# Moving the pooled normalisation of five units to GpSimd in an attention and two-layer MLP kernel, with two roundings and eight feature sums made at other units

## What is computed

```python
# q, k, v: (4, 8, 576, 64)
q_d = q.reshape(B, H, 144, 4, D).mean(axis=3)        # k_d and v_d likewise: the pooled branch
out_d = softmax(scale * q_d @ k_d.T) @ v_d            # 144 x 144 per head
out_up = np.repeat(out_d, 4, axis=2)
mask = np.abs(pos[:, None] - pos[None, :]) < 4        # the band branch
out_local = softmax(where(mask, scale * q @ k.T, -1e9)) @ v
x = (out_up + out_local) -> (2304, 512)
h = x @ w_in;  x = (h * sigmoid(h)) @ w_out           # 512 -> 2048 -> 512
h = x @ w_in2; out = (h * sigmoid(1.702 * h)) @ w_out2
```

## Time and profile before

| | |
|---|---|
| median of 3 runs | 814.86 us (814.63 to 815.61) |
| the profiled execution | 815.39 us, its span 813.6 us |
| TensorE busy | 801.9 us, 99% of the span |
| VectorE, ScalarE, GpSimd busy | 654.1, 538.8, 192.5 us |
| granted TensorE clock | 1.000, full speed (2.4 GHz) |

### The profile page before, as it was taken

The page is one execution under the profiler, slowest core; times in us unless marked ns, Lnnn a source line. Parts: engine busy times, 40 slices in busy tenths (PEclk is TensorE's granted clock), DMA queues, the critical chain, the costliest instruction groups (busy, mean ns, idle before and its releaser), DMA issues.

```text
span 813.6 us, 15682 instructions
## 1 busy us (share of the span) xinstructions
PE 801.9 (99%) x5800; PEld 776.5 (95%) x5800; DVE 654.1 (80%) x944; ACT 538.8 (66%) x865; POOL 192.5 (24%) x199
## 2 busy tenths in 40 slices
PE   9999899999999999999999999999999999999998
PEld 5777699999999999999999999999999999999998
DVE  7999889999998767998768888899655688555466
ACT  5889776578745677655678555677455687455773
POOL 5789786720045420235300000000000000000000
PEclk9999999999999999999999999999999999999999
DMA  7887668776868797677887777878887778877873
GB/s 241 230 253 226 162 198 276 256 284 218 287 209 275 262 322 249 210 264 252 277 292 249 231 253 253 270 234 272 283 289 253 266 252 265 301 251 262 279 254 137
DMA packets 98331, 205.42 MB, mean 252 GB/s; under 512 B 8432, under 2 KB 56048, under 8 KB 98256
## 3 DMA queue, kind: packets, MB, share of 16 engines
q1 hardware_dynamic: 98256, 204.42, 76.5%
HBM read 160.87 MB, written 43.52 MB: 251 GB/s over the span
## 4 chain that ended last, share of the span: by engine, by line
PE 81%; POOL 8%; DVE 7%; issue 4%; ACT 0%; POOLq 0%; DVEq 0%; ACTq 0%
PE hid L330 42%; PE yp L356 36%; DVE gr L547 2%; POOL vpair L980 2%; POOL pband L974 2%; DVE wh L302 2%; POOL vavg L984 1%; PE yp L372 1%; DVE xs L257 1%; POOL G L1005 1%; POOL G L1004 1%; POOL G L1008 1%; PE pt L1183 0%; POOL G L1010 0%; POOL x L271 0%
## 5 line engine op out<-in xcount | busy, mean ns | idle before, releaser
L330 PE MATMUL hid<-xs,wh 128*128 128x384 f32 x2016 | 351.5, 334 | 1.3 <-DVE hw L516 0.8
L330 PEld LDWEIGHTS hid<-xs,wh 128*128 128x128 f32 x2016 | 349.4, 188 | 2.5 <-issue 2.0
L356 PE MATMUL yp<-gr,wh 128*128 128x384 f32 x1968 | 342.1, 334 | 0.0
L356 PEld LDWEIGHTS yp<-gr,wh 128*128 128x128 f32 x1968 | 341.2, 188 | 0.0
L293 ACT ACTIVATE wh<-wr 128x1024 fp32r<-128x1024 f32 (+1 forms) x164 | 164.6, 1003 | 151.4 <-PE hid L330 121.3
L547 DVE TENSOR_TENSOR gr<-G,gr 128x768 fp32r<-128x768 f32 x144 | 137.9, 964 | 52.6 <-ACT gr L428 52.6
L428 ACT ACTIVATE gr<-G 128x768 fp32r<-128x768 f32 x144 | 121.8, 846 | 66.8 <-PE yp L356 66.8
L302 DVE TENSOR_TENSOR wh<-wr,wh 128x1024 fp32r<-128x1024 f32 x76 | 89.9, 1182 | 15.4 <-ACT wh L293 15.1
L391 ACT ACTIVATE G<-G 128x1152 f32<-128x1152 f32 x48 | 55.7, 1161 | 1.1 <-DVE G L542 1.1
L511 DVE TENSOR_TENSOR hv<-p,hid 128x384 f32<-128x384 f32 x48 | 26.3, 548 | 29.2 <-PE hid L330 29.2
L537 DVE TENSOR_TENSOR G<-hv,hid 128x384 f32<-128x384 f32 x48 | 26.4, 550 | 29.1 <-PE hid L330 28.8
(11 more groups left out here) (101 smaller groups left out, 782.7 us busy)
## 6 DMA issues: line engine op xcount, KB each, us to landing
wh<-rests SPq DMA_DIRECT2D x72, 512.0 KB, 3.8
wr<-sums_out SPq DMA_DIRECT2D x48, 512.0 KB, 4.8
wr<-in_w_out SPq DMA_DIRECT2D x36, 512.0 KB, 5.4
rests<-wh SPq DMA_DIRECT2D x36, 512.0 KB, 3.4
wr<-sums_in SPq DMA_DIRECT2D x40, 384.0 KB, 4.0
wr<-in_w_in SPq DMA_DIRECT2D x40, 256.0 KB, 3.6
qk<-in_qkT SPq DMA_DIRECT2D x11, 576.0 KB, 7.1
G<-in_w_in SPq DMA_DIRECT2D x12, 512.0 KB, 5.5
```

The lines of the kernel that those rows point to most:

```text
L330: last = eng.matmul(hid[:, at, 0:HALF], lhsT=wh[:, w % SLOTS, part, a % 4, cc * P:(cc + 1) * P], rhs=xs[:, rest, q, cc, :], start=start an ...
L356: last = eng.matmul(yp[:, at + m, 0:HALF], lhsT=wh[:, w % SLOTS, part, p % 4, m * P:(m + 1) * P], rhs=gr[:, p, rest, :], start=start and p ...
```

## The change

The pooled probabilities of units 1 to 5 are normalised by one GpSimd instruction right behind the band normalisation, after a wait for `a_rcp`; ScalarE leaves its three instructions out there, and keeps them in the other units. The weight batches 0, 1 and 2 are rounded at units 4, 6 and 8 (before: 7, 10 and 12). All eight halves of feature sums are made one unit sooner (6 to 13 in place of 7 to 14). ScalarE copies both pooled groups of transposes in one instruction, after the second one.

```diff
-    ROUNDED_W = {7: 0, 10: 1, 12: 2}
+    ROUNDED_W = {4: 0, 6: 1, 8: 2}
+
+    POOLED = range(1, 6)
...
-    SUMMED = {7: (T1, 0), 8: (T1, 1), 9: (T3, 0), 10: (T3, 1), 11: (T2, 0), 12: (T2, 1), 13: (T4, 0), 14: (T4, 1)}
+    SUMMED = {6: (T1, 0), 7: (T1, 1), 8: (T3, 0), 9: (T3, 1), 10: (T2, 0), 11: (T2, 1), 12: (T4, 0), 13: (T4, 1)}
...
                                   ALU.mult).then_inc(b_nrm, 1)
+                if u.n in POOLED:
+                    eng.wait_ge(a_rcp, u.n + 1)
+                    e = pavg[u.odd]
+                    eng.tensor_tensor(e[:], e[:], rca[:].unsqueeze(2).broadcast_to([AR, NA, SD]),
+                                      ALU.mult).then_inc(a_nrm, NA)
                 eng.wait_ge(vn_in, DMA_INC * (u.n + 1))
...
-                else:
-                    eng.activation(pta[0:HP, j - NLG, :], pt[bank][0:HP, 0:NA * AR],
-                                   ACT.Copy).then_inc(p_cp, 1)
+                elif j == NG - 1:
+
+                    eng.activation(pta[0:HP], pt2[0:HP, :, 0:NA * AR], ACT.Copy).then_inc(p_cp, 2)
...
-                if last is not None and u.n:
+                if last is not None and u.n and u.n not in POOLED:
                     normalise(u)
```

## The result

The changed kernel took 818.4 us in the median of 13 runs (815.83 to 820.39), the kernel before 814.86 us (814.41 to 816.6, 13 runs beside it). The ratio is 1.003, interval 1.0018 to 1.0043: slower by 0.3%. On a second chip the same pair stood at 817.41 and 816.13 us, ratio 1.001 (0.9993 to 1.0028). The forecast of 815.7 had the sign, but 818.4 lies outside its range of 813.3 to 817.2. Both kernels spread over several microseconds, so all that follows rests on medians of about 12 runs each (6 in e11 and e12), and on means with their intervals where two experiments are compared.

The account below looks back on a forecast made before the run. TensorE was taken to bound the attention stage up to iteration 7, then GpSimd's chain. Only the late values of unit 6 added time, all other terms 0: 814.86 + 0.8 = 815.7 us, range 813.3 to 817.2.

Parts of the forecast that it names:

- Where the bound lies: Attention stage: TensorE bounds iterations 1 to 7, GpSimd from 61.04 us; its chain from 56.09 sets the matrix stage's start.
- step 1: Units 1 to 5: taking 5 x 1.03 us off ScalarE is worth 0, as TensorE sets the pace there.
- Price of the inserted instruction: GpSimd's pooled normalisation in units 1 to 5 takes 0.90 us, upper end 1.1, plus 0.18 us of added wait.
- The late values of unit 6: GpSimd in unit 6 waits for values issued later, behind a delayed `v_half`; costs 0.8 us (0 to 1.2).
- Part 2: Feature sums one unit sooner on GpSimd, units 6 to 13: cost 0, at most 0.2 us gained.
- Rival 1: Units 4 and 6: VectorE's rests lose their slot to GpSimd's sums; 1.4 to 2.3 us, middle 1.9, so 816.8; chance 0.20.
- the very sign that was named for this rival: A row of VectorE's early rest (L257) near 32 or 45 us taking more than 1.2 us.
- moves together: From unit 7 on everything shifts alike; the argument against better-falling timing that would give 812.8 us, chance 0.10.
- The rule on who goes first: VectorE and GpSimd on shared SBUF ports: the first to issue holds them for its whole instruction, the other blocks fully.
- Part 3 and 4: Roundings at units 4, 6, 8: 0, up to 0.2 us lost; single copy: 0, at most 0.1 either way per unit.

Follow-up runs that it names:

- e11: Light kernel before the change, with VectorE's early rests (units 4 to 14) as same-size reductions with one SBUF operand instead of two; 811.09 us.
- e12: Changed kernel with loads of queries and keys of units 3 to 15 left out and VectorE's early rests as one-operand reductions of the same size; 810.69 us.
- e1: Kernel before with only the pooled normalisation of units 1 to 5 moved to GpSimd; 816.47 us beside 816.24, ratio 1.0002.
- e5: Changed kernel once more, unaltered, on the second chip; 817.41 us beside 816.13 for the kernel before, ratio 1.001.
- e6: Changed kernel with the pooled part undone, ScalarE normalising all units again; 817.35 us beside 816.13 for the kernel before, ratio 1.0008.
- e2: Kernel before with only the eight feature sums made one unit sooner; 818.33 us beside 816.24, ratio 1.0019.
- e4: Changed kernel with two buffers for the values, so their loads are issued a unit sooner; 817.89 us, ratio 1.0023 to the kernel before.
- e8: Changed kernel with the loads of queries and keys of units 3 to 15 left out; 815.81 us.
- e9: Light kernel before the change with only the pooled normalisation of units 1 to 5 moved to GpSimd; 814.48 us.
- the light kernel: Kernel before with the loads of queries and keys of units 3 to 15 left out; 813.51 us.

## Why the prediction was right or wrong

**Where the bound lies: right.** The matrix stage took the same time (707.5 and 707.7 us from its first product to the end), nearly the whole loss stands before it, and from iteration 1 to 4 the band transposes still came 5.94 to 5.97 us apart. ScalarE's 5 us brought nothing, as step 1 said.

**Price of the inserted instruction: right.** 0.90 forecast, 0.91 measured; the added wait was 0.3 in four units, where I had 0.18, and none in unit 5.

**The late values of unit 6: mechanism there, weight wrong.** The issue moved, and the profiled execution waited 1.96 us where I had put 0.8 with 1.2 as upper bound. The bound failed because I took the landing seen before (at most 5.47 us) for a property of the load; in other profiles in which unit 6 waited for it, it took 4.9 (e1), 5.3 (e5), 6.0 (e6) and 7.2 us (e2). But it is not the main cause of the loss: e4 removed all such waits and stayed slow, and in e8 there were almost none. That the pooled part alone cost 0.7 +- 0.9 us (e1) and 0.8 +- 0.6 (e9), as the 0.8 forecast, is luck: e9's profile has no wait for values at all.

**Part 2, valued at 0: this step failed.** I counted the feature sums on GpSimd's chain from unit 7 to 13 (seven before, seven after), put the cost at 0 and stopped there. Alone it costs 1.7 +- 1.0 us at full load and 1.2 +- 0.8 in the light kernel. GpSimd enters unit 7 without its 0.82 us of slack, its sums stand in another phase to VectorE's rests, and in the profiles the rests lose their turn more often. With the collisions taken away, all parts together cost -0.5 +- 0.7 us (e12 less e11). What failed is this zero: the term left out the time that VectorE and GpSimd take from each other.

**Rival 1: the right cause in too small a frame.** Rests and sums excluding each other is what costs. I worked it out for units 4 and 6 and the pooled part only, at 1.9 us in all, and gave it 0.20. It happened there too (32.90, the rest of unit 4, the very sign that was named for this rival; at 45.78, for the rest of unit 6, GpSimd gave way, as the forecast had assumed). But 13 of the 15 long rests counted above are in units 8 to 14, where I had assumed that everything "moves together", and meetings already cost the kernel before some 2 us in the light form (2.4, own chip 1.8). The row at 96.30 was a sample of that, and the sum gave it no price.

**The rule on who goes first** (the Trainium skill, "SBUF — State Buffer", Who interferes with whom: the loser fully blocks, and issue order decides). Full blocking is what the rows show: 1.88, 2.44, 2.56 us. The order of starts in the trace doesn't decide it: 0.23 us behind GpSimd's start VectorE won at 69.59, 0.21 behind it lost at 57.44 in e8. At 32.90 it even waited for a sum that started after it (33.23). A start in the trace need not be the moment that counts for that rule, so the rule isn't refuted, but no outcome can be read off with it. Such a meeting is to be priced as a chance.

**Part 3 and 4: right as far as seen.** The single copy took 0.73 us for 0.77. The changed kernel:

```profile
46.06 0.73 ACT L1039 ACTIVATE pta<-pt 72x672 f32<-72x672 f32 x1
```

No experiment has them alone. e12, which contains them, is not slower than e11 (-0.5 +- 0.7), and e6, which has them with the sums, not slower than e2 (1.1 and 1.7 us over before).

**Two readings of the rows were off**, without weight for the sum. The band transposes at 29.82 and 36.22 were 6.40 us apart, not 6.0, and GpSimd has six instructions in unit 7, not seven.

**Base.** The medians of the first three runs (814.86) were good for the kernel before on the first chip. On the others its executions spread from 812.6 to 821.2 us, so 0.2% as a threshold was about one standard deviation of single runs.

## What to carry over

When work is moved to GpSimd, or only to another unit there, list the VectorE instructions with two SBUF operands that may run at the same time, and price each new meeting in both outcomes: a microsecond on one engine or the other, and idle time behind. Where several GpSimd instructions follow each other without a wait, a VectorE instruction may have to wait for more than one, so slack ahead of it has a value even on an engine that isn't the bound. To test such a cause, replace the operand and keep the size: a stand-in that doesn't collide (no GpSimd sum was stretched beside it) showed in one pair what ten runs had left open.

## What the runs showed beyond that

A VectorE instruction caught by GpSimd can wait not for one but for two GpSimd instructions in a row (2.56 instead of 1.22 us in unit 7 of e8, 2.44 instead of 0.95 at 96.30). And the landing of one load is no constant: the values of unit 6, issued in the same place of the program, took between 4.9 and 7.2 us from issue to reader in the profiles of the changed kernel, e1, e2, e5 and e6, which all waited for them. Leaving out 40% of the attention stage's loaded bytes (576 of about 1435 KB per unit) gained 2.6 us and more than halved the spread; through which waits isn't shown.
